# Soft mixture-of-experts on one core: gathering peaks and sums over the batches on TensorE in place of GpSimd, and the row softmax behind the slot inputs

## The reference

```
logits = x @ phi                                   # [2304, 32], 8 experts of 4 slots
d = exp(logits - logits.max(0)); d /= d.sum(0) + 1e-9   # softmax over the tokens
slot_input = d.T @ x                               # [32, 512]
for e in range(8): slot_out[e] = relu(slot_input[e] @ w1[e]) @ w2[e]
c = exp(logits - logits.max(1)); c /= c.sum(1) + 1e-9   # softmax over the slots, by row
y = c @ slot_out
... rmsnorm(y), gate and value matmuls, silu(gate) * value @ w_out
```

## Time and profile before

| | |
|---|---|
| median of 3 runs | 820.52 us (820.22 to 822.13) |
| the profiled execution's own time | 822.02 us |
| its span, first to last instruction | 820.0 us |
| busy share of the span | PE 97%, PEld 74%, DVE 61%, ACT 56%, POOL 22% |
| mean granted TensorE clock | 0.99 of 2.4 GHz |
| attention, up to about | 549 us |
| logits to slot inputs | 549 to 580 us |
| experts | 580 to 620 us |
| feed-forward | 620 to 820 us |

### The profile page before, as it was taken

One profiled execution on the slowest core, in us unless ns is written; L12 is line 12 of the kernel. 1 busy time (PEld: TensorE's weight loads), 2 busy tenths in 40 slices (PEclk: granted clock), 3 DMA queues, 4 the chain that ended last, 5 costly groups with the idle time before them and its releaser, 6 DMA issues. The chain is left out here.

```text
span 820.0 us, 17518 instructions
## 1 busy us (share of the span) xinstructions
PE 795.1 (97%) x5858; PEld 606.6 (74%) x5858; DVE 497.2 (61%) x968; ACT 462.4 (56%) x889; POOL 182.9 (22%) x246
## 2 busy tenths in 40 slices
PE   8999999999999999999999999998799999999997
PEld 7777777777777777777777777765334788888886
DVE  6666657657566666665765766743323566666665
ACT  5676666767666667666676766642123453343333
POOL 4541331513315225133151330000002330000000
PEclk9999999999999999999999999999799899999999
DMA  5738856374382553734637417639799001010110
GB/s 150 182 80 260 225 122 158 78 169 105 96 197 63 143 124 85 194 86 116 158 78 166 107 39 198 255 112 394 301 393 392 5 1 52 0 52 1 51 52 26
DMA packets 83033, 112.05 MB, mean 137 GB/s; under 512 B 45360, under 2 KB 47408, under 8 KB 82480
## 3 DMA queue, kind: packets, MB, share of 16 engines
q1 hardware_dynamic: 82832, 111.24, 47.6%
q10 hardware_dynamic: 160, 0.26, 0.1%
HBM read 71.37 MB, written 4.72 MB: 93 GB/s over the span
## 5 line engine op out<-in xcount | busy, mean ns | idle before, releaser
L562 PE MATMUL scores<-k_stack,q_stack 128*128 128x384 f32 x960 | 275.1, 376 | 2.3 <-DVE q_stack L777 1.2
L499 PE MATMUL tbank<-ident,probs 128*128 128x128 f32 x1296 | 219.6, 278 | 2.8 <-DVE pt L868 2.4
L746 ACT COPY pt<-tbank 128x384 f32<-128x384 f32 x256 | 122.7, 479 | 143.9 <-PE tbank L499 142.7
L499 PEld LDWEIGHTS tbank<-ident,probs 128*128 128x128 f32 x1296 | 156.4, 140 | 58.7 <-issue 40.4
L718 ACT ACTIVATE probs<-scores,neg_max 128x1152 f32<-128x1152 f32 x144 | 175.9, 1221 | 6.5 <-PE tbank L499 2.1
L813 DVE TENSOR_REDUCE row_max<-scores 128x1 f32<-128x384 f32 x144 | 80.0, 556 | 130.1 <-PE scores L562 128.2
L562 PEld LDWEIGHTS scores<-k_stack,q_stack 128*128 128x128 f32 x960 | 147.9, 191 | 3.7 <-ACT k_stack L372 1.6
L599 PE MATMUL obank<-pt,v_in 128*64 128x256 f32 x1152 | 148.8, 389 | 0.0
L806 DVE TENSOR_REDUCE row_max<-scores 128x1 f32<-128x768 f32 x144 | 136.7, 949 | 4.4 <-PE scores L562 1.7
L599 PEld LDWEIGHTS obank<-pt,v_in 128*64 128x64 f32 x1152 | 72.8, 136 | 49.3 <-issue 23.5
L337 POOL TENSOR_TENSOR k_hi<-k_lo,one 128x512 fp32r<-128x512 f32 (+1 forms) x45 | 37.2, 826 | 291.4 <-ACT k_lo L670 270.8
(11 more groups left out here) (220 smaller groups left out, 773.6 us busy)
## 6 DMA issues: line engine op xcount, KB each, us to landing
weights<-in_moe_w SPq DMA_DIRECT2D x7, 2048.0 KB, 9.4
v_in<-in_v SPq DMA_DIRECT2D x16, 576.0 KB, 3.9
k_in<-in_k SPq DMA_DIRECT2D x30, 288.0 KB, 4.8
k_stack<-k_hi SPq DMA_DIRECT2D x30, 288.0 KB, 3.7
k_stack<-k_lo SPq DMA_DIRECT2D x30, 288.0 KB, 3.6
q_in<-in_q SPq DMA_DIRECT2D x15, 512.0 KB, 4.7
slots_of_four<-in_moe_w SPq DMA_DIRECT2D x12, 512.0 KB, 11.2
q_stack<-q_hi SPq DMA_DIRECT2D x30, 144.0 KB, 3.3
```

The costliest lines, as they stand in the source:

```text
L499: last = nc.tensor.transpose(tbank[:, bank, cols], src, ident[0:rows, 0:rows])
L562: last = nc.tensor.matmul(scores[:, bank, 0:CH], q_stack[at.par][:, h, order, cols], k_stack[at.par][:, h, keys], start=(x == 0), stop=(x ...
L746: nc.scalar.copy(pt_out(at, e), tbank[:, bank_of(at, e), 0:3 * P].rearrange("p (r q) -> p r q", r=3)).then_inc(out_by_act, 1)
```

## The change

Two constants are built with the logits: `row_group` (which batch a partition belongs to, moved up from `build_spread`) and `same_slot` (128x128, one where two partitions have the same slot). A matmul of `same_slot` with `peak_by` (the peaks, each in the column of its batch) puts all four peaks on every partition, and one with `weight` the sum of the four. The sum now divides `factor` before the fold, so `slot_in` is a plain copy. GpSimd's memset of `slot_in` goes to DVE. The logits' transposes, the row softmax and `build_spread` move behind the slot inputs.

```diff
-    col_a = mem.sb("col_a", [P, NS], FP32)
...
+    peak_by = mem.sb("peak_by", [P, B], FP32)
+    same_slot = mem.sb("same_slot", [P, P], FP32)
...
+    top_ps, total_ps = banks[:, 2, 0:B], banks[:, 0, 0:1]
...
@@ slots_tensor @@
-        for _ in range(2):
+        def keep_busy():
             nc.tensor.matmul(banks[:, NTB - 1, :], ident[:], x_nat[:, 0:NF * P], start=True, stop=True)
+        keep_busy()
+        pe.wait_ge(peak_spread, 1)
+        nc.tensor.matmul(top_ps, same_slot[:], peak_by[:], start=True, stop=True).then_inc(top_ready, 1)
+        keep_busy()
...
-            if i == 1:
-                pe.wait_ge(lt_out, 1)
-                for n in range(NI):
-                    last = nc.tensor.transpose(l_ps[0:rows_of(n), P * n:P * n + P],
-                                               logit_t[:, P * n:P * n + rows_of(n)], ident[:])
-                last.then_inc(l_ready, 1)
+            if i == 0:
+                pe.wait_ge(weight_done, 1)
+                nc.tensor.matmul(total_ps, same_slot[:], weight[:], start=True, stop=True).then_inc(total_ready, 1)
         last.then_inc(z_ready, 1)
+        pe.wait_ge(lt_out, 1)
+        logit_transposes(range(0, 3))
         pe.wait_ge(fold_done, 1)
...
         last.then_inc(s_ready, 1)
+        logit_transposes(range(3, NI)).then_inc(l_ready, 1)
@@ slots_scalar @@
+        act.wait_ge(gap_done, 1)
+        nc.scalar.activation(factor[:], gap[:], ACT.Exp).then_inc(factor_done, 1)
         act.wait_ge(e_ready, 2)
...
-        act.wait_ge(gap_done, 1)
-        nc.scalar.activation(factor[:], gap[:], ACT.Exp).then_inc(factor_done, 1)
-        act.wait_ge(row_shifted, 1)
-        nc.scalar.activation(comb[:], comb[:], ACT.Exp).then_inc(row_exp, 1)
         act.wait_ge(z_ready, 1)
         for half in range(2):
             nc.scalar.copy(z_sum[:, at], z_ps[:, at]).then_inc(z_out, 1)
+        act.wait_ge(row_shifted, 1)
+        nc.scalar.activation(comb[:], comb[:], ACT.Exp).then_inc(row_exp, 1)
@@ slots_gpsimd @@
-        nc.gpsimd.memset(slot_in[:], 0.0).then_inc(slots_clear, 1)
-        pool.wait_ge(col_max, 1)
-        nc.gpsimd.partition_all_reduce(col_b[:], col_a[:], P, ReduceOp.max).then_inc(col_all, 1)
-        pool.wait_ge(col_sum, 1)
-        nc.gpsimd.partition_all_reduce(col_b[:], col_a[:], P, ReduceOp.add).then_inc(col_all, 1)
@@ slots_vector @@
+            if n == 1:
+                nc.vector.tensor_reduce(row_group[:], ident[:, :].rearrange("p (b s) -> p b s", b=B), axis=AX.X, op=ALU.add)
+                then(nc.vector.tensor_copy(same_slot[:, :].rearrange("p (b s) -> p b s", b=B),
+                                           fold[:, :].unsqueeze(1).broadcast_to([P, B, NS])))
...
+        nc.vector.tensor_scalar(peak_by[:], row_group[:], peak[:, 0:1], None, ALU.mult).then_inc(peak_spread, 1)
+        dve.wait_ge(top_ready, 1)
+        then(nc.vector.tensor_reduce(top[:], top_ps, axis=AX.X, op=ALU.max))
+        nc.vector.tensor_tensor(gap[:], peak[:], top[:], ALU.subtract).then_inc(gap_done, 1)
...
+        dve.wait_ge(factor_done, 1)
+        nc.vector.tensor_tensor(weight[:], factor[:], exp_sum[:], ALU.mult).then_inc(weight_done, 1)
         nc.vector.tensor_copy(logit_t[:], lt_ps).then_inc(lt_out, 1)
+        dve.wait_ge(total_ready, 1)
+        then(nc.vector.tensor_scalar(total[:], total_ps, EPS, None, ALU.add))
+        then(nc.vector.reciprocal(total[:], total[:]))
+        then(nc.vector.tensor_tensor(coef[:], factor[:], total[:], ALU.mult))
+        nc.vector.tensor_scalar(fold_f[:], fold[:], coef[:, 0:1], None, ALU.mult).then_inc(fold_done, 1)
+        nc.vector.memset(slot_in[:], 0.0).then_inc(slots_clear, 1)
         dve.wait_ge(s_ready, 1)
         dve.wait_ge(slots_clear, 1)
+        nc.vector.tensor_copy(slot_in[:, :, :, 0:SPE],
+                              s_ps[:, 0:KT * NS].rearrange("p (c e s) -> p c e s", c=KT, e=E)).then_inc(slots_done, 1)
+    def row_shares(dve):
+        dve.wait_ge(l_ready, 1)
+        nc.vector.tensor_reduce(tok_a[:], lflat, axis=AX.X, op=ALU.max).then_inc(row_step, 1)
...
+                                ALU.subtract).then_inc(row_shifted, 1)
+        build_spread(dve)
+        dve.wait_ge(row_exp, 1)
+        nc.vector.tensor_reduce(tok_a[:], cflat, axis=AX.X, op=ALU.add).then_inc(row_step, 1)
...
```

More of the change, by code:

```diff
@@ L933, in rest @@
     mem.at = third + 3 * 4 * F1 + 4 * NI * B * NS
-    col_a = mem.sb("col_a", [P, NS], FP32)
-    col_b = mem.sb("col_b", [P, NS], FP32)
-    picked = mem.sb("picked", [P, NS], FP32)
     fold_f = mem.sb("fold_f", [P, NS], FP32)
-    peak, minus_peak, top, gap, factor, weight, exp_sum = [
-        mem.sb(name, [P, 1], FP32) for name in ("peak", "minus_peak", "top", "gap", "factor", "weight", "exp_sum")]
+    peak_by = mem.sb("peak_by", [P, B], FP32)
+    peak, minus_peak, top, gap, factor, weight, exp_sum, total, coef = [
+        mem.sb(name, [P, 1], FP32) for name in ("peak", "minus_peak", "top", "gap", "factor", "weight", "exp_sum",
+                                                "total", "coef")]
     assert mem.at <= end_r3
@@ L957, in rest @@
     fold = mem.sb("fold", [P, NS], FP32)
-    lowest = mem.sb("lowest", [P, NS], FP32)
+    row_group = mem.sb("row_group", [P, B], FP32)
     mem.at = mem.x_end - 4 * NPAIR * NI * P
@@ L972, in rest @@
     product = mem.sb("product", [P, NI * P], FP32)
-    row_group = mem.sb("row_group", [P, B], FP32)
     row_tile = mem.sb("row_tile", [NI * B, NI], FP32)
@@ L999, in rest @@
     step, row_shifted, row_exp = sem("step"), sem("row_shifted"), sem("row_exp")
-    col_max, col_sum, col_all = sem("col_max"), sem("col_sum"), sem("col_all")
+    row_step = sem("row_step")
+    peak_spread, top_ready = sem("peak_spread"), sem("top_ready")
+    weight_done, total_ready = sem("weight_done"), sem("total_ready")
     gap_done, factor_done, fold_done = sem("gap_done"), sem("factor_done"), sem("fold_done")
@@ L1078, in slots_tensor, with logit_transposes @@
                                         tile_position=(0, 32 * b))
-            if i == 1:
-                pe.wait_ge(lt_out, 1)
-                for n in range(NI):
-                    last = nc.tensor.transpose(l_ps[0:rows_of(n), P * n:P * n + P],
-                                               logit_t[:, P * n:P * n + rows_of(n)], ident[:])
-                last.then_inc(l_ready, 1)
-        last.then_inc(z_ready, 1)
+            if i == 0:
+                pe.wait_ge(weight_done, 1)
+                nc.tensor.matmul(total_ps, same_slot[:], weight[:], start=True, stop=True).then_inc(total_ready, 1)
+        last.then_inc(z_ready, 1)
+        def logit_transposes(tiles):
+            for n in tiles:
+                last = nc.tensor.transpose(l_ps[0:rows_of(n), P * n:P * n + P],
+                                           logit_t[:, P * n:P * n + rows_of(n)], ident[:])
+            return last
+        pe.wait_ge(lt_out, 1)
+        logit_transposes(range(0, 3))
         pe.wait_ge(fold_done, 1)
@@ L1147, in slots_vector @@
         then(nc.vector.memset(high_mask[96:128, :], 0.0))
-        then(nc.vector.tensor_scalar(lowest[:], fold[:], -1.0, -NEG, ALU.add, ALU.mult))
         for n in range(1, len(xt_jobs), 2):
             xt_job_out(dve, nc.vector.tensor_copy, n).then_inc(xt_out_v, 1)
+            if n == 1:
+                nc.vector.tensor_reduce(row_group[:], ident[:, :].rearrange("p (b s) -> p b s", b=B), axis=AX.X, op=ALU.add)
+                then(nc.vector.tensor_copy(same_slot[:, :].rearrange("p (b s) -> p b s", b=B),
+                                           fold[:, :].unsqueeze(1).broadcast_to([P, B, NS])))
         dve.wait_ge(lt_step, NI)
@@ L1159, in slots_vector @@
                               ).then_inc(e_out_v, 1)
+        dve.wait_ge(factor_done, 1)
+        nc.vector.tensor_tensor(weight[:], factor[:], exp_sum[:], ALU.mult).then_inc(weight_done, 1)
         nc.vector.tensor_copy(logit_t[:], lt_ps).then_inc(lt_out, 1)
-        then(nc.vector.tensor_scalar(picked[:], fold[:], peak[:, 0:1], None, ALU.mult))
-        nc.vector.tensor_tensor(col_a[:], picked[:], lowest[:], ALU.add).then_inc(col_max, 1)
+        dve.wait_ge(total_ready, 1)
[4 more added lines that the diff above has]
+        nc.vector.memset(slot_in[:], 0.0).then_inc(slots_clear, 1)
+        dve.wait_ge(s_ready, 1)
+        dve.wait_ge(slots_clear, 1)
+        nc.vector.tensor_copy(slot_in[:, :, :, 0:SPE],
+                              s_ps[:, 0:KT * NS].rearrange("p (c e s) -> p c e s", c=KT, e=E)).then_inc(slots_done, 1)
+    def row_shares(dve):
         cflat = comb[:, :, :, :].rearrange("p i b s -> p (i b) s")
@@ L1166, in slots_vector @@
         dve.wait_ge(l_ready, 1)
[L1167 to L1171, removed]
+        nc.vector.tensor_reduce(tok_a[:], lflat, axis=AX.X, op=ALU.max).then_inc(row_step, 1)
+        dve.wait_ge(row_step, 1)
@@ L1172, in slots_vector @@
         nc.vector.tensor_tensor(cflat, lflat, tok_a[:, :].unsqueeze(2).broadcast_to([P, NI * B, NS]),
```

(15 more changed lines are left out.)

4 lines of the change are left out of this document (removed).

## The result

| | before | changed |
|---|---|---|
| median of the runs, us | 820.89 (820.22 to 822.13, 4 runs) | 815.48 (814.75 to 816.15, 4 runs) |
| profiled execution, us | 822.02 | 814.84 |
| its span, us | 820.0 | 812.8 |
| its mean granted clock | 0.990 | 1.000 |

The ratio is 0.9926, with a 95% interval of 0.9906 to 0.9945: 5.4 us faster, at a forecast of 815.5.

A forecast was written before the change was run, and what follows sets the result against it. GpSimd's late start delayed the fold, and TensorE then met the value-weight loads at share(1, 3). The lesser gain, the DMA's 4.9 plus 0.1 slack, gave 820.5 - 5.0 = 815.5 us; range 812.5 to 818.8.

The forecast's parts named there:

- The place that decides: Start of share(1, 3) on TensorE (S): TensorE and value-weight loads arrive 0.1 us apart; TensorE's extra gain becomes waiting.
- Sum: At share(1, 3): lesser of TensorE's 5.8 to 9.3 us and the DMA's 4.9 plus 0.1 slack, so 5.0 us.
- End of the weighted sums: Two new matmuls against five transposes gone from ahead of it: net 0 us, bounds -0.8 to +0.8.
- Copies and fold: Copies to z_sum no longer wait for late work; experts start at 573.2 or 574.1, 5.8 to 6.7 us earlier.
- First w1 pass: Experts' first w1 matmuls: 9.66 us before, 7.0 at full clock; 2.6 us to win if the clock holds.
- Moves with no price: Row softmax, build_spread and same_slot work in their new places: hidden, with the row work done by 579.9.
- The DMA: Hole in the loads from 578 to 586 us closes, worth 4.9 us; value weights land at 624.2.
- the second stretch at half clock: From 636.2 to 643.3 us, costing 1.4; may vanish (-1.4) or last 5.5 us over busy work (+1.3).
- A: Rival, 20%: clock falls among TensorE's new waits between value weights, adding some 2.7 us: 818.2, at most 821.0.
- B: Rival, 10%: loads don't bind at share(1, 3), TensorE's 9.3 us comes through: 811.2, or 813 with part.
- C: Rival, 5%: the wait changes its name, the fold waiting for fold_done or the peaks' matmul delaying exponentials: 817.9.
- D: Rival, 4%, slower: TensorE at half clock from the first value weight well into the dense matmuls: 822.3, up to 824.

The follow-up runs named there:

- e1: Changed kernel plus twelve needless fp32 matmuls on TensorE behind the first w1 pass, ahead of the value weights: 815.93 us, ratio 0.9932 to the kernel before.
- e2: Changed kernel with the loads behind the first quarter of the first w1 pass held until that pass ends: 818.19 us, ratio 0.9961.
- e6: Changed kernel with w2's rows laid out so each partition reads longer pieces, hidden-layer transposes reordered to match: 815.42 us, ratio 0.9929.
- e0: The changed kernel run again, unaltered: 816.86 us, ratio 0.9942 to the kernel before.
- e3: Changed kernel with the row softmax back ahead of the slot inputs, so the matmul gathers alone: 816.0 us, ratio 0.9932.
- e11: The changed kernel run a third time, unaltered, on another chip: 815.86 us, ratio 0.9937 to the kernel before.
- e5: Changed kernel plus twelve needless fp32 matmuls on TensorE right behind share(1, 3): 819.5 us, ratio 0.9975 to the kernel before.
- e9: Changed kernel with w2 read in longer pieces and the small g_sb load moved behind the second group's first w1 load: 814.98 us, ratio 0.9921.
- e10: Changed kernel with longer w2 pieces, the later g_sb load and three filler matmuls in TensorE's w_low wait behind share(1, 3): 814.22 us, ratio 0.9915.
- e4: Kernel before, gathers still on GpSimd, with the row exponential behind the z_sum copies and the row subtraction behind slot_in: 820.33 us, ratio 0.9987.

## Why the prediction was right, point by point

**The place that decides** was named right, by the landing time of the value weights in the earlier trace rows: S waits for its loads in every run with the gathers on TensorE, e1 shows that TensorE's lead is idle there, e2 and e6 that S moves when the loads do. *Sum*: 5.0 forecast, 4.9, 5.3 and 4.7 measured at S, and 5.4, 4.8 and 4.7 in the medians. That the first median meets 815.5 to the tenth is luck: two of its four executions held the clock behind S (814.8) and two did not (816.1 and 816.2), and it lies between them.

**End of the weighted sums**: 0 forecast (-0.8 to +0.8). SP's L1024 comes 21.93 us from the block's start, where L1022 came 21.64: +0.3; in e0 it comes at 21.65, so +0.0. The matmul of the peaks was ready later than forecast: `peak_by` came at 564.52, and its weight load waited 0.97 us.

**Copies and fold**: 573.2 forecast for the experts with the clock held, 573.98 measured, or 6.4 us earlier as counted from the block's start (5.8 to 6.7 forecast). The fold took 1.05 (1.0 forecast), and the clock held through it. **First w1 pass**: 7.07 (7.0). With the 2.6 won there TensorE's lead is 9.0, at the upper end of 5.8 to 9.3. Of that, 9.0 - 4.9 = 4.1 had to turn into waits (up to 4.3 forecast); the profile shows 3.3 of it as waits for DMA, and the other 0.8 not as waits. The sign asked for 3 to 4 us at the value weights; 1.8 lie there and 1.5 earlier, at the last quarter of w2.

**Moves with no price**: the memset took 0.91 us on DVE (bounds 0.17 and 1.4) and was over at 570.19, ahead of the fold. The row softmax was over at 579.1 (579.9 forecast), ahead of the experts' copy that comes next on DVE. Hidden both, and e3 shows that even the place of the row softmax is worth nothing that can be measured here.

**The DMA**: 407 GB/s stand where the hole was. By the issue and landing times the last value weight lands 75.0 us from the block's start (605.4 + 19.7 - 550.1) instead of 79.5 (609.3 + 19.8 - 549.55): 4.5 earlier (4.9 in e0 and 4.3 in e11), where 4.9 was forecast. The slack of 0.1 was read from the weight load; the matmuls of `share(1, 3)` started 0.3 behind that load before and with it after. So the slack was 0.4, and the hole in this execution worth 0.4 less than forecast: the two errors cancel.

**What was mis-sized** is the second stretch at half clock, priced at 1.4 us if it vanishes. Where it vanished, S to D is 1.7 us shorter than before and D to the end 1.2: 2.9 in all. The prediction counted only the dense work from 640.4 on and took what lies ahead of it to be free; from 636.2 to 640.4 most of it is TensorE's work too. In 12 of the 16 executions the mean clock is under 1.000, so the medians of e0 and e11 show little of this.

**The rivals.** A: the clock did fall in most executions, but behind S, where it had fallen before as well, not in the bursts between the value weights (1.00 from 586 to 630). The Trainium skill (TensorE: Matmul & The Clock Gate, HAM oscillation) tells of waits for DMA, longer than the bursts of work between them, that send the clock back to half each time. The traces don't bear this out for waits as short as the 0.75 and 1.03 us here, between bursts of 0.85; after the one of 3.1 us in e2 the clock fell. B fell with e1, C with the fold's start 0.5 us behind the copies, D with all of these.

## What to carry to other kernels

A wait of 6.4 us on the busiest engine was worth 5, because a second chain, the loads, ended 0.1 us ahead of it. Ask of the place where two chains meet what the slower of them wins, and take the smaller gain; then see whether needless work on the engine costs time ahead of that place and behind it (e1, e5), which tells in two runs what binds. Where a chain of loads binds, look first for stretches in which the queue ran dry because an issue waited for compute; and when the loads ahead of such an issue get shorter, look there again (e9).

## What the runs showed of the hardware that was not expected

The granted clock behind S differs between executions of one kernel: from 631 to 638 us it was 1.00 in one and 0.52 in another, with 5.20 and 5.27 us of TensorE work from 624 to 631, and 0.51 in e10 after 6.90. It is worth up to 2.9 us, and what decides it stays open.

With each partition's rows of w2 lying together, the stretch from 586 to 606 us, most of which is loads of w2, moved 408 instead of 386 GB/s (e6).

GpSimd stood idle for 8.01 and 7.30 us ahead of its first gather in both kernels that use it there (before and e4), without a wait that the profile shows; the second gather had no such delay.
